# Attention state scan with a mixer and a channel mix: where the second batch splits the weights of the channel-down product

## The reference

```python
for t in range(S):
    state = alpha[:, :, t, :, None] * state + np.einsum('bhd,bhe->bhde', k[:, :, t], v[:, :, t])
    y[:, :, t] = np.einsum('bhd,bhde->bhe', q[:, :, t], state)
...
h = np.maximum(xt @ w_tok1, 0.0) @ w_tok2            # 768 -> 256 -> 768 over the tokens
u = x + h.transpose(0, 2, 1)
x = u + np.maximum(u @ w_ch1, 0.0) @ w_ch2           # 384 -> 1536 -> 384 over the channels
...
k = np.maximum(xk @ w_k, 0.0);  v = k * k @ w_v      # 384 -> 1024 -> 384
r = 1.0 / (1.0 + np.exp(-(xr @ w_r)));  out = r * v  # xk, xr mix x with the token before
```

## Time and profile before

| | |
|---|---|
| median of 3 runs | 740.62 us (740.38 to 740.81) |
| profiled execution, its own time | 741.02 us |
| its span | 739.3 us |
| busy: TensorE, its weight loads, VectorE, ScalarE, GpSimd | 731.8, 724.0, 461.5, 330.7, 196.9 us |
| granted TensorE clock, share of full speed | 1.00 |

### The profile page before, as it was taken

The page is one execution under the profiler, slowest core; times in us unless marked ns, Lnnn a source line. Parts: engine busy times, 40 slices in busy tenths (PEclk is TensorE's granted clock), DMA queues, the critical chain, the costliest instruction groups (busy, mean ns, idle before and its releaser), DMA issues.

```text
span 739.3 us, 13805 instructions
## 1 busy us (share of the span) xinstructions
PE 731.8 (99%) x4598; PEld 724.0 (98%) x4598; DVE 461.5 (62%) x1279; ACT 330.7 (45%) x943; POOL 196.9 (27%) x344
## 2 busy tenths in 40 slices
PE   8999999999999999999999999999999999999998
PEld 7899999999999999999999999999999999999998
DVE  6988878764877873787874312446356374473661
ACT  4865644442544442444443232335455373363551
POOL 2874545341224442233534340320000000000000
DMA  9974433431424331243330024010011010110000
GB/s 198 209 143 95 91 50 68 58 40 41 53 38 58 74 48 25 58 54 45 77 73 1 33 79 145 33 33 34 33 44 53 32 33 32 53 43 32 11 21 32
DMA packets 174042, 43.82 MB, mean 59 GB/s; under 512 B 161312, under 2 KB 171168, under 8 KB 173984
## 3 DMA queue, kind: packets, MB, share of 16 engines
q1 hardware_dynamic: 170736, 37.98, 25.8%
q0 software_dynamic: 1152, 4.72, 1.7%
q10 hardware_dynamic: 2096, 0.39, 0.3%
HBM read 33.63 MB, written 9.44 MB: 58 GB/s over the span
## 4 chain that ended last, share of the span: by engine, by line
PE 94%; DVE 2%; ACT 2%; issue 1%; DMA 1%; SPq 0%; DVEq 0%
PE bank L742 21%; PE bank L758 20%; PE bank L835 14%; PE bank L813 14%; PE bank L822 5%; PE bank L659 4%; PE bank L627 3%; PE bank L730 3%; PE bank L698 3%; PE bank L664 2%; PE bank L657 2%; PE bank L721 1%; PE bank L622 1%; PE bank L635 1%; PE bank L710 1%; ACT x_half L914 1%
## 5 line engine op out<-in xcount | busy, mean ns | idle before, releaser
L920 ACT ACTIVATE hid_hi<-bank 128x384 fp32r<-128x384 f32 x96 | 47.2, 492 | 118.2 <-PE bank L742 118.2
L1177 DVE SCALAR_TENSOR_TENSOR hid_lo<-bank,hid_hi 128x384 fp32r<-128x384 f32 x96 | 53.3, 555 | 68.1 <-ACT hid_hi L920 67.0
L1022 ACT ACTIVATE relu_k<-bank 128x384 f32<-128x384 f32 x64 | 31.4, 491 | 106.0 <-PE bank L813 86.2
L742 PE MATMUL bank<-u_hi,wch_hi 128*128 128x384 f32 x288 | 72.2, 358 | 0.0
L742 PE MATMUL bank<-u_lo,wch_hi 128*128 128x384 f32 x288 | 66.3, 338 | 0.0
L758 PE MATMUL bank<-hid_lo,wch_hi 128*128 128x384 f32 x288 | 65.5, 335 | 0.0
L742 PE MATMUL bank<-u_hi,wch_lo 128*128 128x384 f32 x288 | 65.5, 334 | 0.0
L758 PE MATMUL bank<-hid_hi,wch_hi 128*128 128x384 f32 x288 | 65.4, 334 | 0.0
L758 PE MATMUL bank<-hid_hi,wch_lo 128*128 128x384 f32 x288 | 65.4, 334 | 0.0
L514 POOL TENSOR_SCALAR_AFFINE_SELECT relu_k<-relu_k 128x256 f32<-128x256 f32 x72 | 29.3, 407 | 124.1 <-ACT relu_k L902 124.1
L1287 DVE TENSOR_TENSOR x_half<-bank,x_half 128x384 f32<-128x384 f32 x24 | 13.4, 557 | 77.5 <-PE bank L835 75.4
(11 more groups left out here) (135 smaller groups left out, 1837.3 us busy)
## 6 DMA issues: line engine op xcount, KB each, us to landing
w_raw<-in_moe_w_ch SPq DMA_DIRECT2D x12, 384.0 KB, 3.6
x_scratch<-x_half POOLq DMA_DIRECT2D x8, 576.0 KB, 3.5
out<-x_half SPq DMA_DIRECT2D x24, 192.0 KB, 1.9
vt<-in_v SPq DMA_DIRECT2D x48, 72.0 KB, 2.2
qka<-in_q SPq DMA_DIRECT2D x49, 48.0 KB, 2.2
qka<-in_alpha SPq DMA_DIRECT2D x49, 48.0 KB, 2.2
qka<-x_scratch SPq DMA_DIRECT2D x4, 577.5 KB, 3.8
qka<-in_k SPq DMA_DIRECT2D x48, 48.0 KB, 2.2
```

Of the source, the lines that this page charges most:

```text
L742: mm = nc.tensor.matmul(dst, ch1_w(a, n % KC, jj), u[c][:, n % KC, half * HT:(half + 1) * HT], start=(n == 0), stop=(n == 3 * KC - 1))
L920: nc.scalar.activation(dst, b_ring[t % 2][:, 0:HT], func).then_inc(tile_hi, 1)
L1177: ins = nc.vector.scalar_tensor_tensor(dst, src, 0.0, hi, ALU.max, ALU.subtract)
```

## The change

GpSimd's twelve halves are placed by a table. With NJ = 12 it reads 1, 1, 3, 5, 6, 7, 8, 9, 10, 11, 12, 13: half 1 comes one slot earlier, half 3 and all after it one slot later, halves 0 and 2 stay. ScalarE splits the first piece in slot 1, behind the copy of scores and ahead of the tile's high part, no longer at the end of slot 0. The other five stay in slots 2, 4, 6, 8 and 10 but stand ahead of `spread_q`, where they stood behind it.

```diff
--- before.py
+++ after.py
@@ -477,6 +477,8 @@
                 nc.gpsimd.tensor_tensor(dst[1][:, off:off + rows * cols], staging(n)[0],
                                         dst[0][:, off:off + rows * cols], ALU.subtract).then_inc(w_lo_ready, 1)
 
+            HALF_SLOT = (1, 1, 3, *range(5, NJ + 2))
+
             def split_half_lo(jj):
 
                 n, half = divmod(jj, 2)
@@ -546,8 +548,9 @@
                 sc, yo, prep = step_in(s, 2), step_in(s, 3), prepared(r, s)
                 if sc is not None:
                     clear_future(r, sc)
-                if r == 1 and 1 <= s <= NJ:
-                    split_half_lo(s - 1)
+                for jj in range(NJ):
+                    if r == 1 and HALF_SLOT[jj] == s:
+                        split_half_lo(jj)
                 if yo is not None and step(r, yo)[0] < NC - 1:
                     own_head(r, yo)
                 if yo is not None and step(r, yo)[1] == NP - 1:
@@ -877,13 +880,15 @@
                     high_x(r, yo)
                 if sc is not None:
                     store_scores(r, sc)
+                if r == 1 and s == 1:
+                    split_hi(CH1_END)
                 if s > 0:
                     tile_first(r - 1, s)
                 tile_second(r - 1, s)
+                if r == 1 and s > 0 and s % 2 == 0 and s < NJ:
+                    split_hi(CH1_END + s // 2)
                 if prep is not None:
                     spread_q(*prep)
-                if r == 1 and s % 2 == 0 and s < NJ:
-                    split_hi(CH1_END + s // 2)
 
             def high_x(r, i):
                 c, p = step(r, i)
```

## The result

Over 22 runs of each, the changed kernel takes 739.54 us in the median (738.99 to 740.59) and the kernel before 740.74 us (740.34 to 741.94). The ratio is 0.9983 with a 95% interval of 0.9977 to 0.9988: 1.20 us faster, where 1.23 us was forecast; the median lies in the forecast range of 739.0 to 740.4. It is a real gain, of 0.17%. The changed kernel's profiled execution took 739.70 us (739.79 was forecast), with a span of 737.9 us, 1.4 us less than that of before.

What follows compares the result with a forecast made beforehand. TensorE bounds the kernel (waits lie on it for 94% of the span), its winnable idle at or just ahead of 68.4 to 76.2 us; -0.46 - 0.31 - 0.46 = -1.23 us gives 739.39 us (profiled 739.79), range 739.0 to 740.4.

Steps and rivals of the forecast that it cites:

- The two stalls: TensorE's waits before the scores of steps 2 and 3, second batch: 0.46 and 0.31 us, plus 0.46 us restarting; all go.
- Who made them late: Slot 3: GpSimd's half holds VectorE's `qs_lo` pair 0.91 us; lateness and then `split_hi` (0.83 us) delay the scores copy.
- The parts set to nothing: Side effects of the moves in slots 1, 8 and 13, bounded at 0.91 or 0.83 us, taken as costing TensorE nothing.
- The second half in slot 1: Two GpSimd halves in a row in slot 1: at worst hold VectorE 0.91 us, taken as 0.
- the push of `spread_q` in slots 8 and 10: Split ahead of `spread_q`: in slot 8 up to 0.83 us pushed on, taken as 0; slot 10's split called off the road.
- the pair of slot 13: Slot 13: a half joins `prepare_x2` and can hold one `qs_lo` by at most 0.91 us; TensorE needs it a slot later.
- Rival 1: Only the first stall goes, with its restart (0.69 us), and a wait comes in slots 5 or 6: 739.93 us; chance 0.16.
- The margin of 0.34 us: Slot 6: `own_head` behind the half ends at 198.16, TensorE wants its state at 198.50 (third-batch time); no stall, thinnest place.
- Rival 2: Nothing goes: the `qs_lo` pair was held by its second `qs_hi`, not by GpSimd; 740.6 us, chance 0.08.
- Rival 3: Half 3's loads, queued behind piece 5, land late and delay TensorE from a landing past 95.7; 741.7 us at 98.0; chance 0.05.
- The price, one for one: Late loads of half 3: each us of landing beyond about 95.7 costs TensorE one us.
- The queue's numbers: Times worked out for the changed kernel: SP's load issue ends 89.3, loads land 91.5, `own_head` margin 0.34, scores copy 72.58.

Runs made afterwards that it cites:

- the extra instructions: Changed kernel plus one extra GpSimd instruction behind split_k in ten slots of the third batch, five kinds by turns; one run took 739.21 us.

## Why the prediction was right, and where it was not

**The two stalls.** Right in size and cause. The wait on `qs_lo` and the one on the scores copy went, with both restarts, 1.23 us in the trace to the hundredth, and nothing was given back up to the end: from unit 0 to the end of the span it is 669.6 us, where it was 670.8. The step that carried it, comparing the stretch with the same code one batch later, turned out stronger than the list of stalls: the two recorded stalls hold 0.77 us, the distance holds all 1.23.

**Who made them late.** Right for GpSimd and `qs_lo`, now shown and not only met together. Both causes that it gave the second stall, VectorE late and `split_hi` in the way, are there; it did not weigh them, and the split is the larger, 0.33 of 0.53 us. The Trainium skill's two sentences come apart as weighed: GPSIMD Engine Reference, section Key points, which counts VectorE instructions with two SBUF inputs among those that contend, agrees with every neighbour here that reads SBUF, and the memset, which does not, ran free; the note in Advanced Engine Details and Errata, section VectorE Performance Modes, names only two-port instructions and leaves out the case that this kernel has. The prediction set that page against the other by this note alone; further down, under GPSIMD Details, the same page names two SBUF inputs too.

**The parts set to nothing.** The second half in slot 1 cost 0 (the `u_lo` beside it took 0.56 us), the push of `spread_q` in slots 8 and 10 cost 0, as did the pair of slot 13. The moves of half 1 and of the splits of slots 0, 2, 6, 8 and 10 brought nothing measurable either. The prediction did not say that most of the diff was idle; it had the means to, since TensorE had holes in slots 4 and 5 alone.

**Rival 1**, a wait in slot 5 or 6 in place of the second stall, did not come: TensorE is full in both. Its mechanism is real, though: with VectorE still late, as in the two kernels that keep a half in slot 4 beside ScalarE's new order, `own_head` of slot 6 made TensorE lose 0.11 us. The margin of 0.34 us was worked out to the end of `own_head`; the 0.14 us or so from there to the start of L660 was not taken off. **Rival 2** fell by the extra instructions, and by ScalarE's edit alone, which left the pair at 1.52 us.

**Rival 3** is the step that failed, though it decided nothing here. The prediction let the lateness reach TensorE only at the scores of step 9, from a landing at 95.7, with 4 us of cover. I followed the turned data forward and forgot what queues behind the turn on VectorE: the state and output of step 6, which `own_head` and TensorE want in the same slot. The point is at 94.2 and the cover 2.5 us. The price, one for one, was too small too (6.0 us for a turn 4.4 us too late), because a hole of 4.2 us takes the clock with it for a while.

**The queue's numbers.** Issue end 89.61 for 89.3, turn at 91.70 for 91.5, margin in slot 6 0.31 for 0.34, scores copy 72.41 for 72.58. All came from shifting the third batch's rows by a constant, which is safe where the same code runs with the same waits.

## What to carry to other kernels

Where a loop body runs twice, once with and once without an extra job, subtract the two stretches: the difference is the most that moving the job can win, and the clean one serves as the timetable of the changed kernel. Place a GpSimd instruction that reads SBUF where VectorE works from PSUM, not beside a VectorE instruction with two SBUF tensors. When a transfer gets later, the cover ends at the first consumer of anything that queues behind the waiting instruction, not at the consumer of the data.

## What the runs showed of the hardware

A GpSimd copy, affine_select or tensor_tensor of 384 columns held a VectorE instruction with two SBUF tensors until it ended (the pair grew from 0.61 to 0.99, 1.00 and 1.51 us); a memset of the same size, which reads nothing, did not (0.61 us). VectorE instructions with a PSUM operand were not seen to be held (`u_lo` took 0.56 us inside a half, and 0.54 to 0.56 us in all its 24 places).

After 4.2 us without a matmul TensorE's granted clock went from 1.00 to 0.50 (2.4 to 1.2 GHz) about 1 us into the work that followed, and was back at 1.00 at 106 us; three matmuls of 384 columns took 1.16 us there, where they take 0.69 in the changed kernel. The stalls of 0.3 to 0.5 us of the kernel before did not lower it.
